# Output products of 128 rows, merged Gram products and another MLP order in a recurrence, mixture-of-experts and MLP kernel

## The reference

```python
# 1: per batch and head (8 heads, 40 channels), a recurrence over 768 steps
y[t]  = r[t] @ state
Sa    = state @ a[t]
state = state * w[t] - outer(Sa, b[t]) + outer(v[t], k[t])
# 2: x = y of all heads side by side (320); 4 experts of causal attention, the top 2 weighted by gates
out  += gate[e] * (softmax(causal(x @ wq[e] @ (x @ wk[e]).T / 8)) @ (x @ wv[e]) @ wo[e])
# 3: MLP with a spatial gate
h = relu(x @ w_in); u, v = h[:, :512], h[:, 512:]
v_n = (v - mean(v)) / sqrt(var(v) + 1e-6)
out = (u * (w_spatial @ v_n + b_spatial)) @ w_out
```

## Time and profile before

| what | value |
|---|---|
| three runs | 1008.78, 1017.11, 1019.47 us (median 1017.11) |
| profiled execution | 1006.58 us, its span 1004.7 us |
| mean granted TensorE clock | 0.991 |
| TensorE busy (matmul) | 956.4 us, 95% of the span |
| VectorE, ScalarE, GpSimd busy | 521.8, 462.3, 238.7 us |
| matmuls | 15708 |

### The profile page before, as it was taken

One profiled execution on the slowest core, in us unless ns is written; L12 is line 12 of the kernel. 1 busy time (PEld: TensorE's weight loads), 2 busy tenths in 40 slices (PEclk: granted clock), 3 DMA queues, 4 the chain that ended last, 5 costly groups with the idle time before them and its releaser, 6 DMA issues.

```text
span 1004.7 us, 36936 instructions
## 1 busy us (share of the span) xinstructions
PE 956.4 (95%) x15708; PEld 687.9 (68%) x15708; DVE 521.8 (52%) x1443; ACT 462.3 (46%) x1122; POOL 238.7 (24%) x344
## 2 busy tenths in 40 slices
PE   6799999999999999989998999999999999999898
PEld 4678888888888888876646655676556665567455
DVE  7677777787787777654344244312443124431210
ACT  6455655665655655643247334443344333343401
POOL 7344444354354444311000001100011000110011
PEclk8899999999999999999999999999999999999999
DMA  4244434354334334251150100001000000000001
GB/s 147 73 112 115 122 106 132 98 153 119 103 97 127 102 100 123 70 140 30 40 175 1 40 0 1 1 34 47 1 1 1 34 8 1 1 1 34 8 1 39
DMA packets 51539, 63.68 MB, mean 63 GB/s; under 512 B 27440, under 2 KB 37488, under 8 KB 51376
## 3 DMA queue, kind: packets, MB, share of 16 engines
q1 hardware_dynamic: 51376, 61.32, 20.8%
HBM read 53.42 MB, written 7.86 MB: 61 GB/s over the span
## 4 chain that ended last, share of the span: by engine, by line
PE 81%; DVE 11%; issue 5%; ACT 3%; DMA 1%; DVEq 0%; ACTq 0%
PE banks L1627 13%; PE banks L662 7%; PE banks L726 6%; PE banks L1567 5%; PE banks L1545 4%; PE banks L1519 4%; PE banks L1596 4%; PE banks L1639 4%; PE banks L1609 4%; PE banks L1579 4%; DVE state_z L1140 4%; PE banks L908 3%; PE banks L898 3%; PE banks L773 3%; PE banks L657 2%
## 5 line engine op out<-in xcount | busy, mean ns | idle before, releaser
L510 ACT ACTIVATE powers_z<-powers,parity 128x256 f32<-128x256 f32 x240 | 108.9, 502 | 165.7 <-DVE powers L1013 165.6
L1390 POOL TENSOR_TENSOR v_st<-v_st,u_t 128x384 f32<-128x384 f32 x32 | 31.9, 998 | 478.5 <-DVE v_st L1779 478.5
L1627 PE MATMUL banks<-w_st,v_n 128*128 128x384 f32 x384 | 140.4, 501 | 4.9 <-issue 4.9
L726 PE MATMUL banks<-pq,powers_z 64*64 64x64 f32 (+1 forms) x3072 | 133.1, 224 | 11.5 <-issue 6.0
L726 PEld LDWEIGHTS banks<-pq,powers_z 64*64 64x64 f32 x3072 | 112.0, 137 | 18.2 <-issue 7.8
L458 POOL TENSOR_TENSOR state<-state_sum,dc 128x160 f32<-128x160 f32 x92 | 68.8, 748 | 175.5 <-DVE state_sum L1126 175.5
L1395 ACT ACTIVATE probs_t<-banks 128x512 f32<-128x512 f32 (+1 forms) x96 | 51.9, 543 | 120.8 <-PE banks L1567 120.7
L1627 PEld LDWEIGHTS banks<-w_st,v_n 128*128 128x128 f32 x384 | 68.3, 192 | 53.5 <-issue 17.4
L1118 DVE SCALAR_TENSOR_TENSOR vu_tok<-banks,minus,vz_tok 128x80 f32<-128x80 f32 x192 | 48.8, 296 | 70.2 <-PE banks L908 70.2
L1725 DVE CUSTOM_DVE_ANT_0 probs<-banks,hide 128x128 f32<-128x128 f32 (+5 forms) x96 | 56.0, 622 | 51.8 <-PE banks L1545 51.4
L1409 ACT ACTIVATE probs<-probs,neg_max 128x128 f32<-128x128 f32 (+5 forms) x96 | 63.5, 662 | 31.3 <-DVE neg_max L1725 31.3
(11 more groups left out here) (165 smaller groups left out, 1809.0 us busy)
## 6 DMA issues: line engine op xcount, KB each, us to landing
w_all<-decays_dram SPq DMA_DIRECT2D x48, 160.0 KB
w_all<-kb_ch_dram SPq DMA_DIRECT2D x48, 160.0 KB
vz_tok<-vz_tok_dram SPq DMA_DIRECT2D x24, 320.0 KB, 3.6
r_all<-rz_ch_dram SPq DMA_DIRECT2D x48, 160.0 KB
x_dram<-y_tok SPq DMA_DIRECT2D x384, 10.0 KB, 2.0
a_raw<-a_ch_dram SPq DMA_DIRECT2D x48, 80.0 KB
vc_tok<-vc_tok_dram SPq DMA_DIRECT2D x24, 160.0 KB, 4.2
r_all<-r_ch_dram SPq DMA_DIRECT2D x48, 80.0 KB
```

What stands on the lines that cost most here:

```text
L510: act.activation(powers_z[:, i, :, j, :], powers[:, i, :, :], ACT.Copy, scale=parity[:, j:j + 1])\
L726: ins = pe.matmul(to[r, k * n:k * n + n], powers_z[r, i, k, :, :].rearrange("p j t -> p (j t)"), right, start=True, stop=True)
L1627: ins = pe.matmul(bank[M_BANK + j % 2][:, 0:TH], v_n[:, i, d * P:d * P + P], w_st[:, i, t], start=(i == 0), stop=(i == BLOCKS - 1))
```

## The change

In the recurrence:

- **Outputs.** `from_values` takes 128 rows at once, both halves `p`, with 80 columns: 16 products per unit instead of 32. For this `kb_tok` gets a fifth index, with zeros where a row's half isn't the product's (GpSimd writes the zeros once; ScalarE's copy of `kb_tok` becomes four instructions of 64 rows instead of two of 128). The output bank is laid out anew (`out_place`), so that a product writes two pieces of 40 elements with 40 between; the inputs r, w and a are reordered outside (`by_outputs`), and the order of channel blocks in `place`. `from_values` now stands beside `from_states`, at (1, 0) and (3, 0).
- **Grams.** One `grams(t)` at (0, 0) with 64 columns of keys per product replaces the two halves. Its outputs for N and for `akz` alternate by 32 columns in the Gram bank. `first_power` masks 512 elements (`n_z`, both parities, with `straight`) and transposes them into `powers_z[0]`, so ScalarE's spread of the first power goes; GpSimd adds the two parities to `n_t` (`n_joined`).
- **Keys.** The new order of blocks makes the scaling of keys by decays eight instructions of 128 elements instead of two of 512.
- **Levels.** Level 0 moves to (2,1) and (2,2); levels 1, 2 and 4 are cut 4 and 4 (before 2 and 6).

In the MLP, VectorE's variance, `inverse_deviation` and the first `normalise` go in among the last four reads of `factors`, and each spatial product of the first piece waits for its own block only.

The diff, cut to its core (constants, semaphores and the twin edits of other engines' waits are left out):

```diff
-            a, p = q // 2, (q % 2) ^ (c & 1)
-            return a, p, 2 * p + 1 - a, c * NC + 2 * p + 1 - a
+            return a, p, 2 * p + 1 - a, c // 2 * 8 + p * 4 + c % 2 * 2 + 1 - a
+        def out_place(c, a):
+            return 2 * (c % 2) + 1 - a, c // 2 * 2
...
             def first_factor(u):
                 pool.wait_ge(n_read, at(u, n_read))
+                if u > 0:
+                    pool.wait_ge(level_ready[0], at(u - 1, level_ready[0]))
+                pool.tensor_tensor(n_t[:, :, :], n_z[:, :, 0, :], n_z[:, :, 1, :], ALU.add).then_inc(n_joined, 1)
+                pool.wait_ge(n_joined, at(u, n_joined))
...
                 for a in range(2):
-                    pool.tensor_tensor(*keys_by_decays(u, a), ALU.mult).then_inc(kb_scaled, 1)
+                    for c in range(NC):
+                        pool.tensor_tensor(*keys_by_decays(u, a, c), ALU.mult).then_inc(kb_scaled, 1)
...
             pool.wait_ge(consts, CONSTS)
+            pool.memset(kb_tok[:, 0], 0.0).then_inc(kb_pads, 1)
             pool.memset(r_all[:, 0:6 * W], 0.0).then_inc(r_pads, 1)
...
-            def grams(u, kind):
+            def grams(u):
+                pe.wait_ge(az_done, at(u, az_done))
+                to = bank[GRAM_BANK].rearrange("p (c x j t) -> p c x j t", x=2, j=2, t=C)
                 for c in range(NC):
                     for q in range(Q):
                         a, p, g, blk = place(c, q)
-                        slot = 1 - a if kind == 0 else a
-                        ins = pe.matmul(bank[GRAM_BANK][rows32(2 * p + slot), col:col + 2 * C],
-                                        kb[:, (a * NC + c) * 2 + p, slot, :],
+                        first = (a * NC + c) * P + p * 2 * C
+                        ins = pe.matmul(to[rows64(p), c, :, 1 - a, :], kb_ch[:, u % 3, first:first + 2 * C],
                                         az_ch[:, blk, :, :], start=True, stop=True)
...
             def level(u, i, low=0, high=N8):
                 if low == 0:
-                    pe.wait_ge(spread[i], at(u, spread[i]))
+                    if i == 0:
+                        pe.wait_ge(turned[0], at(u, turned[0]))
+                        pe.wait_ge(n_joined, at(u, n_joined))
+                        pe.wait_ge(akz_read, at(u, akz_read))
+                    else:
+                        pe.wait_ge(spread[i], at(u, spread[i]))
...
             def from_values(w, first):
-                for c in range(first, first + 2):
-                    for x in range(2):
-                        for q in range(Q):
-                            a, p, g, blk = place(c, q)
-                            col = c * X + x * D
-                            pe.matmul(bank[Y_BANK][rows32(g), col:col + D], rvu[rows64(p), c * 2 + a, x, :],
-                                      kb_tok[rows64(p), w % 3, a, c, x, :], start=False, stop=(c < 2),
+                to = bank[Y_BANK][:, 0:NC * X].rearrange("p (k x d) -> p k x d", x=2, d=D)
+                for x in range(2):
+                    for c in range(first, first + 2):
+                        for a in range(2):
+                            g, k = out_place(c, a)
+                            pe.matmul(to[rows32(g), k:k + 2, x, :], rvu[:, c * 2 + a, x, :],
+                                      kb_tok[:, w % 3, a, c, x, :, :], start=False, stop=(c < 2), skip_group_check=True)
...
-                if (c, j) == (0, 1):
-                    if valid(x):
-                        from_values(x, 2)
-                    if valid(v):
-                        pe.wait_ge(d_read, at(v, d_read))
-                        level(v, 1, 0, 2)
+                if (c, j) == (0, 1) and valid(v):
+                    pe.wait_ge(d_read, at(v, d_read))
+                    level(v, 1, 0, 4)
...
                     if valid(x):
                         pe.wait_ge(state_n_read, at(x, state_n_read))
+                        from_values(x, 2)
                         from_states(x, 2)
                 if (c, j) == (1, 1):
-                    if valid(t):
-                        level(t, 0, 0, 4)
                     if valid(v):
-                        level(v, 2, 0, 2)
+                        level(v, 2, 0, 4)
...
                 if (c, j) == (2, 0):
-                    if valid(t):
-                        grams(t, 1)
...
                 if (c, j) == (2, 1):
                     if valid(t):
-                        level(t, 0, 4, N8)
+                        level(t, 0, 0, 4)
...
-                if (c, j) == (2, 2) and valid(v):
-                    level(v, 3, 2, N8)
+                if (c, j) == (2, 2):
+                    if valid(v):
+                        level(v, 3, 2, N8)
+                    if valid(t):
+                        level(t, 0, 4, N8)
...
                         from_states(w, 0)
-                if (c, j) == (3, 1):
-                    if valid(w):
                         from_values(w, 0)
...
             def first_power(u):
-                dve.tensor_tensor(n_t[:, :, :], bank[GRAM_BANK][:, 0:N8 * C].rearrange("p (k t) -> p k t", t=C),
-                                  upper[:, 0, :].unsqueeze(1).to_broadcast([P, N8, C]), ALU.mult).then_inc(n_read, 1)
+                from_grams(u, n_z[:, :, :, :], straight).then_inc(n_read, 1)
                 dve.wait_ge(n_read, at(u, n_read))
-                turn_power(u, 0, n_t[:, :, :])
+                dve.transpose(powers_z[:, 0].rearrange("p k j t -> p (k j) t"),
+                              n_z[:, :, :, :].rearrange("p k j t -> p (k j) t")).then_inc(turned[0], 1)
...
                         if x == 0:
                             pe.wait_ge(w_late, W_LATE)
-                            pe.wait_ge(v_normed, at(m, v_normed, BLOCKS))
+                        if j == 0:
+                            pe.wait_ge(v_normed, at(m, v_normed, i + 1))
...
+                        if j == 2 * DT - 4:
+                            variance(m)
+                        if j == 2 * DT - 3:
+                            inverse_deviation(m)
+                        if j == 2 * DT - 2:
+                            normalise(0)
-                    for i in range(BLOCKS):
+                    for i in range(1, BLOCKS):
                         normalise(i)
```

More of the change, by code:

```diff
@@ L151, in recurrence @@
         turned = [sem("turned%d" % i, 1) for i in range(LEVELS)]
[L152 removed]
+        spread = [None] + [sem("spread%d" % i, 2) for i in range(1, LEVELS)]
         level_ready = [sem("level_ready%d" % i, 1) for i in range(LEVELS)]
@@ L490, in _ @@
                     scaled_a(u + 3)
+                if u == 0:
+                    for i in range(1, 3):
+                        pool.memset(kb_tok[:, i], 0.0).then_inc(kb_pads, 1)
                 if valid(u):
@@ L778, in from_states @@
             def from_states(w, first):
-                for c in range(first, first + 2):
-                    for q in range(Q):
-                        a, p, g, blk = place(c, q)
-                        ins = pe.matmul(bank[Y_BANK][rows32(g), c * X:c * X + X], r_ch[:, w % 2, cols(blk)],
-                                        state_n[:, c, q, :, :], start=(c == 0), stop=(c >= 2), skip_group_check=True)
+                for b in range(2):
+                    for c in range(first, first + 2):
+                        for a in range(2):
+                            q = 2 * a + b
+                            _, p, _, blk = place(c, q)
+                            g, k = out_place(c, a)
+                            ins = pe.matmul(bank[Y_BANK][rows32(g), (k + p) * X:(k + p) * X + X], r_ch[:, w % 2, cols(blk)],
+                                            state_n[:, c, q, :, :], start=(c < 2 and b == 0), stop=(c >= 2),
+                                            skip_group_check=True)
                 if first == 2:
@@ L943, in _ @@
             level(0, 2)
-            first_grams(1)
+            grams(1)
             level(0, 3)
-            level(1, 0, 0, 4)
-            grams(1, 1)
+            level(1, 0)
             level(0, 4)
-            pe.wait_ge(akz_read, at(1, akz_read))
-            level(1, 0, 4, N8)
             for u in range(UNITS + 2):
@@ L1006, in scaled_first @@
                 for a in range(2):
-                    dve.tensor_tensor(*keys_by_decays(0, a), ALU.mult).then_inc(kb_scaled, 1)
+                    for c in range(NC):
+                        dve.tensor_tensor(*keys_by_decays(0, a, c), ALU.mult).then_inc(kb_scaled, 1)
             def turn_power(u, i, src):
@@ L1904, in channels, with by_outputs @@
         return np.moveaxis(x, -1, 2).reshape(U, 2, D, -1)
-    r, k, v, w, a, b = (blocks(inputs[name]) for name in ("r", "k", "v", "w", "a", "b"))
+    def by_outputs(x):
+        return x.reshape(U, 2, 2, 2, 2, 2, C, D).transpose(0, 1, 2, 4, 3, 5, 6, 7).reshape(x.shape)
+    k, v, b = (blocks(inputs[name]) for name in ("k", "v", "b"))
+    r, w, a = (by_outputs(blocks(inputs[name])) for name in ("r", "w", "a"))
     zero = np.zeros_like(w[..., :1, :])
```

127 lines of the change are left out of this document (62 added, 65 removed).

## The result

| | before | after |
|---|---|---|
| runs, median | 1008.78 to 1019.47, 1013.49 us (4 runs) | 1029.54 to 1040.20, 1033.89 us (4 runs) |
| ratio | 1 | 1.0202, 95% interval 1.0148 to 1.0255 |
| profiled execution, its span | 1006.58, 1004.7 us | 1040.20, 1038.4 us |
| mean granted TensorE clock in it | 0.991 | 0.970 |
| matmuls | 15708 | 14172 |

A forecast was written before the change was run, and what follows sets the result against it. VectorE was taken to bound u-to-g stretches and TensorE g-to-u stretches. Recurrence +38, prologue +3 and MLP -6 us gave +35 on a 1013 us mean: 1048 us, range 1024 to 1064 (8 in 10).

The forecast's parts named there:

- Two kinds of stretch: Recurrence hops: VectorE sets u product to next g (2.49 us, TensorE's fill free); TensorE sets g to u.
- rival 1: TensorE bounds the kernel throughout, so removing two islands of matmuls gains: 1002 us; chance 9%.
- from_values, +0.58: Output products at (1,0) and (3,0): removed islands gain 0, two added groups of 16 matmuls cost +0.58 us per unit.
- Grams, +0.18: Merged Gram products: (0,0) grows by 0.63 us, (2,0) shrinks by 0.45, so +0.18 us per unit.
- first_power and state_z, +0.45: Hop 0, VectorE: larger mask and transpose add 0.55 us, state_z gives back 0.10; +0.45 us per unit.
- so I take a third of it: Hop 0: only a third of state_z's possible saving is realised, -0.10 us, bounds 0 and -0.30.
- rival 2: Cheaper Grams at the old pace, or state_z freed in full: 1036 to 1043 us; chance 12%.
- Level 0 at (2,2), +0.37: Sixteen more TensorE matmuls at (2,2) cost 0.49 us less 0.12 slack: +0.37 per unit, bounds 0.2 and 0.5.
- Sum: Recurrence terms together: +1.58 us per unit, +38 us for 24 units.
- Prologue, +3: Start: first level 0 waits for GpSimd's joined N, until 17.1 us; +3 us, bounds 1 and 6.
- MLP, -6: Last round after the last block: spatial products start earlier, less low clock; -6 us, bounds -3 and -7.
- Rival 3, strided outputs: PSUM writes in pieces with gaps double the streams of both new products: 1081 us; chance 6%.

The follow-up runs named there:

- e2: Changed kernel with from_values moved back to its old places, (0,1) and (3,1); 1023.86 us, ratio 1.0101.
- e4: Kernel before with from_values left out, so outputs lack the values' part; 1009.50 us, ratio 0.9960.
- e11: Kernel before, unchanged, profiled once more to see how two executions differ; 1015.43 us.
- e1: Kernel before with only the MLP part of the change; 1010.65 us, ratio 0.9952.
- e3: Changed kernel with VectorE's first_power at (0,0), ahead of vu_tok, instead of (0,1); 1030.30 us, ratio 1.0181.
- e12: e9 with the Grams merged as in the change, n_z and its transpose at (0,0), level 0 at (2,1) and (2,2); 1012.74 us, 0.9975.
- e8: e5 with late GpSimd key products, from_values in its old places, first_power's mask at (0,0) and transpose at (0,1); 1005.03 us, ratio 0.9912.
- e6: e3 with GpSimd's key products in two halves, moved out of the first hop; 1024.37 us, ratio 1.0063.
- e9: e8 with levels 1 and 4 cut after two of eight parts again, as in the kernel before; 996.32 us, ratio 0.9822.
- e10: Kernel before with only GpSimd's two key products issued later, away from hop 0's state_z; 1006.84 us, ratio 0.9920.
- e5: Kernel before with the new from_values, its eight key products, levels 1 and 4 cut 4 and 4, and the MLP part; old Grams; 1016.73 us, 1.0003.
- e7: Changed kernel with GpSimd's start reordered, n_t's join ahead of the zeros and unit 1's keys; 1033.23 us, ratio 1.0144.

## Why the prediction came out as it did

It said 1048 us, 1024 to 1064, slower with 0.85; 1033.9 was measured, slower by 2.0% (+20.4 us for +35). The mechanism was right; one term was sized wrong, and one thing was left out of the sum.

- **Two kinds of stretch.** Right. VectorE's stretches are 2.49 us with (e2, but for the 0.10 of its cut) and without (e4) their fill; rival 1 is out. The changes of tile shape that e4 takes out with the fill give nothing there either.
- **from_values, +0.58.** 1.99 and 1.83 measured for 2.00 and 1.84 predicted, +0.55. Right, and so was the 0.29 for 16 matmuls (0.30).
- **Grams, +0.18.** (0,0) 2.58 for 2.57, (2,0) 2.22 for 2.21. Right.
- **first_power and state_z, +0.45.** Measured +0.24, u-g 3.12 for 3.3. n_z (0.68 for 0.69) and the transpose (0.71 for 0.72) were as sized; the failing step is "so I take a third of it": state_z fell in full from 0.79 to 0.49 (-0.30 for -0.10), since the longer chain puts its start 0.12 us ahead of kb_ch's end (243.81 against 243.93), within the 0.15 us that aren't held, although kb_ch takes 0.84 us more. That is the half of rival 2 that came true; its cheap Grams did not.
- **Level 0 at (2,2), +0.37.** Measured +0.47 in (2,1) and (2,2) together, the upper bound: (2,1) became 0.04 longer too.
- **Sum.** +1.454 for +1.58 us per unit, +34.9 for +38.
- **Prologue, +3.** Level 0 at 18.48 us for 17.1, the first g 4.9 us later than on the page and 2.7 later than in e11. Too small was "about 1 us" for what precedes kb_ch: it starts at 13.98, and the pieces take 3.72 us, not 2.9. Behind it units 0 and 1 run at a lower clock for longer.
- **MLP, -6.** -6.0 in e1; -3.8 in the changed kernel's own profiled execution. Right in size.
- **Rival 3, strided outputs.** Out: L828 writes 40 of 80 elements in 0.30 us for 16 as L815 does without gaps, L710 writes 32 of 64 in the 1.08 us of L801. The rule of the Trainium skill that stood for it (PSUM — Partial Sum Buffer, Specifications (TRN2)) shows no effect here.
- **What was left out.** "The other units repeat it, plus scattered waits of some tenths": I carried the scattered waits over as they were. They are 7 to 11 us in the two executions of before and 2.5 in the changed kernel's (0.2 in e3). From e11 to the changed kernel the ledger reads +2.7 (first g) +33.4 (hops) -8.5 (scattered) +1.4 (low clock and ends) -4.2 (MLP) = +24.8.
- **How much of it is luck.** From the page's execution, on which the sum was made, the ledger reads +4.9 +33.4 -4.7 +3.8 -3.8 = +33.7, nearly the forecast's 35, but with errors that cancel: the scattered waits against the start and the clock. The medians differ by 20.4 only, since the page's execution lies 6.9 us below before's median and the changed kernel's 6.3 above its own. The latter fits its clock (0.970, the other three 0.979 to 0.985): over the 25 runs of before beside e1, 0.01 of granted clock goes with 5 us. The former wasn't separated further.

**What stays open.** Whether the slower use of instructions is all of what the merged form spares: e4 speaks against their number alone, since it has 14172 matmuls like the changed kernel and keeps 7.8 us, and no run moved the places of the packets. Nor does the load of the DMA queues explain who pauses: during the pauses between 70 and 420 us their mean share is 0.29 in the page's execution and 0.45 in e11, against 0.40 and 0.39 over the whole stretch. In unit 9 of e12 the packet set out only 0.5 us before the pause began, which is why the pause is long; why it set out so late wasn't separated, nor why the clock fell behind 1.60 us in e8 and not behind 1.59 in the changed kernel.

## What to carry to other kernels

First sort the gaps of a chain by what ends them: if their length doesn't follow their fill, they are free room, and moving work out of them into a gap that TensorE sets costs all of its time, however much leaner the work has become. When an instruction leaves the path, ask what is late next: here a state_z held by GpSimd and a state product queued behind a level took what the move of 1.39 us of VectorE work should have given; e6 frees the one, e9 both. Compare hops, not whole spans, and keep scattered waits and the clock as terms of their own, since two executions of one kernel differ by 9 us and two versions of it by little more. For a pause that the profile puts to nobody, look at the queue that brings the instructions.

## What the runs showed of the hardware that I had not expected

- A GpSimd product that is off the path holds VectorE's state_z, for as long as the one instruction has left (less 0.15 us): 0.49 us alone, mostly 0.79 and once 1.62 in before. The profile shows a longer instruction, not a wait. Moving the product alone gained 0.8% (e10).
- Writes to PSUM in pieces of 32 or 40 elements with gaps of the same length cost nothing that shows here.
- GpSimd's pieces of 128 elements take 0.42 us each (3.35 for eight), those of 512 take 1.25: a quarter of the work costs a third.
- TensorE pauses for 0.3 to 2.2 us, at times in the middle of equal matmuls, at one fixed instruction of each packet of 256, and goes on 1.2 to 1.7 us behind a packet's landing: it waits for instructions. In e2, e5, e7, e8 and e12 the granted clock was at its lower level (0.5, 1.2 GHz) for 7 to 14 us around or behind such a pause, and in e12 that cost more than the pause.
